# Key-value products of six batches in wider tiles, and fewer filler products, in a soft-MoE kernel over linear attention

## The reference

```python
kv  = einsum('bhsd,bhse->bhde', k, v)             # per batch and head: 64x64
out = einsum('bhsd,bhde->bhse', q, kv)
x   = out / sqrt(mean(out*out, -1) + 1e-6) * g_norm   # then (4608, 512)
logits = x @ phi                                   # (4608, 32)
d = exp(logits - logits.max(0)); d /= d.sum(0) + 1e-9
slot_input = (d.T @ x)                             # 32 slots
slot_out[e] = relu(slot_input[e] @ w1[e]) @ w2[e]  # w1: 512x1024, w2: 1024x512
c = exp(logits - logits.max(1)); c /= c.sum(1) + 1e-9
return c @ slot_out                                # (4608, 512)
```

## Time and profile before

| | |
|---|---|
| median of the runs | 171.85 us |
| profiled execution, its span | 172.24 us, 170.8 us |
| TensorE busy | 148.4 us (87%), 1821 matmuls and as many weight loads |
| VectorE, ScalarE, GpSimd busy | 85.7, 89.0, 60.6 us |
| DMA | 71.65 MB, 419 GB/s over the span |
| mean granted clock of TensorE | 0.975 of full speed |

### The profile page before, as it was taken

How to read it: one execution, slowest core, us unless ns; L and a number is a source line. 1 busy time by engine, 2 the same in 40 slices (tenths; PEclk the granted TensorE clock), 3 DMA queues, 4 the chain that set the end, 5 groups by cost and what they waited for, 6 DMA issues and landing times.

```text
span 170.8 us, 4205 instructions
## 1 busy us (share of the span) xinstructions
PE 148.4 (87%) x1821; PEld 103.4 (61%) x1821; DVE 85.7 (50%) x184; ACT 89.0 (52%) x232; POOL 60.6 (36%) x76
## 2 busy tenths in 40 slices
PE   7978998979999999999899998899989799988100
PEld 3547887969767878797697673366557443445000
DVE  1111437743669166762946698636885046229100
ACT  3114778795887686859749866213221044328100
POOL 7000246757177735477382678700000004000000
PEclk9999999999999999999999999999999999999955
DMA  5999999999999999999899999999999989999995
GB/s 183 436 450 407 482 411 419 430 502 414 414 405 468 414 444 479 418 429 418 384 420 465 460 426 395 470 412 387 418 430 445 455 387 414 429 413 430 423 452 236
DMA packets 3357, 71.65 MB, mean 419 GB/s; under 512 B 678, under 2 KB 678, under 8 KB 810
## 3 DMA queue, kind: packets, MB, share of 16 engines
q1 hardware_dynamic: 2986, 71.18, 97.4%
q0 software_dynamic: 352, 0.20, 0.4%
HBM read 61.94 MB, written 9.44 MB: 418 GB/s over the span
## 4 chain that ended last, share of the span: by engine, by line
PE 43%; DMA 31%; ACT 10%; DVE 6%; SPq 1%; issue 1%
PE psum L205 43%; DMA arena<-in_kv_dram 20%; DMA arena<-in_w_dram 11%; ACT bd L205 3%; ACT sq L205 2%; ACT arena L205 2%; DVE ms L205 2%; DVE logits L205 1%; SPq L205 1%; ACT part L205 1%; ACT d L205 1%; DVE part L205 1%; ACT r L205 1%; DVE acc L205 0%; DVE r L205 0%
## 5 line engine op out<-in xcount | busy, mean ns | idle before, releaser
L205 PE MATMUL psum<-bd,arena 128*128 128x192 f32 (+1 forms) x320 | 56.8, 336 | 2.2 <-ACT arena L205 1.0
L205 PEld LDWEIGHTS psum<-bd,arena 128*128 128x128 f32 (+1 forms) x320 | 45.5, 179 | 10.5 <-ACT arena L205 3.5
L205 PE MATMUL psum<-arena 128*64 128x64 f32 (+2 forms) x896 | 36.0, 270 | 2.9 <-DMA arena<-in_kv_dram 1.8
L205 DVE TENSOR_REDUCE ms<-sq 128x16 f32<-128x1024 f32 (+1 forms) x19 | 22.0, 1162 | 29.9 <-ACT sq L205 29.7
L205 PEld LDWEIGHTS psum<-arena 128*64 128x64 f32 (+2 forms) x896 | 27.5, 129 | 13.8 <-issue 4.1
L205 POOL TENSOR_TENSOR part<-part,r 128x512 f32<-128x512 f32 x17 | 17.8, 1047 | 49.7 <-DVE r L205 49.7
L205 POOL TENSOR_TENSOR arena<-arena,r 128x512 f32<-128x512 f32 x34 | 34.7, 1042 | 0.0
L205 ACT COPY arena<-psum 128x512 f32<-128x512 f32 (+2 forms) x48 | 30.8, 651 | 7.1 <-PE psum L205 7.1
L205 ACT ACTIVATE sq<-psum 128x512 f32<-128x512 f32 x36 | 21.5, 596 | 9.5 <-PE psum L205 9.3
L205 ACT COPY part<-psum 128x256 f32<-128x256 f32 (+1 forms) x38 | 13.7, 360 | 10.5 <-DVE part L205 9.3
L205 DVE TENSOR_REDUCE logits<-part 128x64 f32<-128x512 f32 (+1 forms) x17 | 17.2, 1013 | 0.0
(11 more groups left out here) (75 smaller groups left out, 103.4 us busy)
## 6 DMA issues: line engine op xcount, KB each, us to landing
arena<-in_kv_dram SPq DMA_DIRECT2D x1, 6912.0 KB, 30.4
arena<-in_t_dram SPq DMA_DIRECT2D x1, 6912.0 KB, 25.2
arena<-in_w_dram SPq DMA_DIRECT2D x1, 6912.0 KB, 28.0
arena<-in_w_dram SPq DMA_DIRECT2D x1, 6144.0 KB, 24.2
arena<-in_w_dram SPq DMA_DIRECT2D x3, 2048.0 KB, 18.8
arena<-in_w_dram SPq DMA_DIRECT2D x1, 5120.0 KB, 18.6
arena<-in_w_dram SPq DMA_DIRECT2D x1, 4352.0 KB, 31.8
arena<-in_w_dram SPq DMA_DIRECT2D x1, 4096.0 KB, 23.3
```

Source lines behind the costliest of these rows:

```text
L205: inst = getattr(engine, method)(*args, **kwargs)
```

## The change

Batches 0 to 4 (`WIDE = 5`) get a PSUM area twice as wide, a 128x128 block for each pair of heads. In batch 0 every product of 128 tokens, and that of the last 64, is taken for two heads at once: one 128x128 matmul in place of two of 64x64, of which the two 64x64 blocks on the diagonal are used. In batches 1 to 4 only the last 64 tokens are taken so, and first (with `start`); the 64x64 products of the main chunks add to the diagonal blocks. `kvT` is then copied in two halves of 64 partitions, for batch 0 one on ScalarE and one on VectorE, for batches 1 to 4 both on ScalarE. Batches 5 to 7 stay. The filler products ahead of the loop go from five products of zeros and two of ones to one and three; in each half of batch 0 one product of zeros goes, and behind the first half there is one of ones in place of two.

```diff
-EARLY = (5, 2, 0)
+EARLY = (1, 1, 0)
...
+WIDE = 5
...
+            if self.wide:
+                half = kv_rest(self.b, g).rearrange("p (w n) -> p w n", w=2)[64 * w : 64 * w + 64]
+                nc.tensor.matmul(
+                    self.pkv[:, w, g], lhsT=half[:, 1], rhs=half[:, 0], start=g == 0 or self.b == 0, stop=False
+                )
             for c in range(4):
+                if self.b == 0:
+                    nc.tensor.matmul(
+                        self.pkv[:, w, g], lhsT=main[:, w, 1, c], rhs=main[:, w, 0, c], start=False, stop=c == 3
+                    )
+                    continue
                 for i in range(2):
                     lo = 64 * i
+                    at = lo if self.wide else 0
                     nc.tensor.matmul(
-                        self.pkv[lo : lo + 64, w, g],
+                        self.pkv[lo : lo + 64, w, g, at : at + 64],
...
-            for g in gs:
+            for g in () if self.wide else gs:
...
-            nc.scalar.copy(self.kvT, self.pkv[:, :, gs[0] : gs[0] + n].rearrange("p w g d -> p g w d"))
+            pkv = self.pkv[:, :, gs[0] : gs[0] + n].rearrange("p w g d -> p g w d")
+            if not self.wide:
+                nc.scalar.copy(self.kvT, pkv)
+                return
+            nc.scalar.copy(self.kvT[:64], pkv[:64, :, :, :64])
+            if self.b:
+                nc.scalar.copy(self.kvT[64:], pkv[64:, :, :, 64:])
+            else:
+                nc.vector.tensor_copy(out=self.kvT[64:], in_=pkv[64:, :, :, 64:])
...
-    fill_wide(ps.tile([P, 512], F32, tag="m", name="fill"), 2)
+    fill_wide(ps.tile([P, 512], F32, tag="m", name="fill"), 3)
...
         kv.borders((g,))
-        fill(1, cols=512)
         kv.slots((g,))
```

More of the change, by code:

```diff
@@ L390, in __init__ @@
             t = ps.tile([P, 2, 512], F32, tag=tag, name=f"kvp{b}_{tag}", bufs=bufs)
-            self.pkv = t[:, :, :128].rearrange("p w (g d) -> p w g d", g=2)
-            self.pT = t[:, 0, 128:384].rearrange("p (g n) -> p g n", g=2)
-            self.pM = t[:, 1, 128:384].rearrange("p (g h w n) -> p g h w n", g=2, h=2, w=2)
+            self.wide = b < WIDE
+            n = 256 if self.wide else 128
+            self.pkv = t[:, :, :n].rearrange("p w (g d) -> p w g d", g=2)
+            self.pT = t[:, 0, n : n + 256].rearrange("p (g n) -> p g n", g=2)
+            self.pM = t[:, 1, n : n + 256].rearrange("p (g h w n) -> p g h w n", g=2, h=2, w=2)
         def products(self, r):
@@ L397, in products @@
             main = kv_main(self.b, g).rearrange("p (r w c n) -> p r w c n", r=2, w=2, c=4)
-            for c in range(4):
+            if self.wide:
[3 more added lines that the diff above has]
+                )
+            for c in range(4):
+                if self.b == 0:
[3 more added lines that the diff above has]
+                    continue
                 for i in range(2):
                     lo = 64 * i
+                    at = lo if self.wide else 0
                     nc.tensor.matmul(
-                        self.pkv[lo : lo + 64, w, g],
+                        self.pkv[lo : lo + 64, w, g, at : at + 64],
                         lhsT=main[:, w, 1, c, lo : lo + 64],
                         rhs=main[:, w, 0, c, lo : lo + 64],
-                        start=c == 0 and (g == 0 or self.b == 0),
-                        stop=False,
+                        start=c == 0 and g == 0 and not self.wide,
+                        stop=self.wide and g == 1 and c == 3,
                     )
         def borders(self, gs):
-            for g in gs:
+            for g in () if self.wide else gs:
                 half = kv_rest(self.b, g).rearrange("p (w n) -> p w n", w=2)
```

## The result

The changed kernel takes 178.91 us (median of 6 runs, 178.43 to 179.39) beside 171.84 of the kernel before on the same chip (171.59 to 171.95): a ratio of 1.0414, interval 1.0393 to 1.0434. The forecast was 171.5. The profiled execution took 179.14 with a span of 177.8, 7.0 more than before. Two executions at a far lower clock, of 191.41 us (kernel before) and 709.93 us (last experiment), are left out of all times, but the fetches of the last experiment are counted in the latter. The wide batches are five, 0 to 4, not six as the title has it.

The account below looks back on a forecast made before the run. The prediction took the last DMA engine to bound the kernel: one fetch fewer gains 0.35 us, TensorE's added time costs nothing, so 171.85 becomes 171.50 us. Forecast 171.35 to 171.65; wider range 171.2 to 171.95.

Parts of the forecast that it names:

- What bounds the kernel: Whole span: DMA engines stream 71.65 MB at 430 GB/s without a hole; the last engine to finish ends the kernel.
- How late could a DMA be: Loads and last store: slack is time from issue to landing less own bytes at 430 GB/s; 8.7, 6.4, 1.6 us.
- 8.7 us to spare: Load of `in_t`, 6912 KB: 25.2 us to landing against 16.5 us for its bytes.
- 6.4 us: Slack of the 5120 KB of weights that tile 35's stage releases: 18.6 us to landing against 12.2 for the bytes.
- 1.6 us for the last store: Slack of the last store, 3072 KB: 4.2 us beyond its bytes, of which some 2.6 are what any DMA pays.
- TensorE's time: Batches 0 to 4: fewer instructions but more TensorE time, 0.85 us per half of batch 0, 0.75 per later batch; costs nothing.
- At most 3.9 us late at the weights' issue: TensorE's delay bound there: up to 2.4 us passed on from batches 0 to 2, plus 1.5 from batches 3 and 4.
- The path of the delay: Batches 0 to 2 add up to 3.2 us; idling before the fourth batch's load takes 0.76; batches 3 and 4 add 1.5.
- Fetches: TensorE's instruction queue: 156 instructions fewer, so the fourteenth 16 KB fetch, at 154.67 us, falls away; gain 0.35 us.
- no gain: Rival, 171.85 us: the fetch is not on the last DMA engine, or comes all the same; chance 0.16.
- Slower: Rival, from 172.2 to 174 us: TensorE late at the last store, 1.4 us at the bound; chance 0.07.
- clock branch: Part of the slower rival: TensorE's clock falls around 10 us with fewer fillers, some 5 us of hole.

Follow-up runs that it names:

- last experiment: Kernel before with five products of ones exchanged for 32 tiny products of zeros each, meant to bring one fetch more (15); 172.07 us, ratio 1.0033.
- delay behind the issue: Kernel before with two more products of ones (1.7 us of TensorE) directly behind the issue of the last weights; 171.75 us, ratio 0.9997.
- batch 0 alone: Changed kernel with only batch 0 wide, batches 1 to 4 as in the kernel before; 171.97 us, ratio 1.0002.
- batches 1 and 2 in one row, tiny products: Batches 0 to 2 wide, wide products grouped, with 32 tiny products of zeros for one product of ones ahead of batch 0; 172.06 us, ratio 1.0013.
- batches 1 and 2 in one row: Changed kernel, batches 0 to 2 wide: wide products of 1 and 2 ahead of the narrow, batch 0's 64-row products side by side; 172.01 us.
- same with zeros thinned: Wide products of batches 1 and 2 grouped as in its parent, with fewer zero products, 32 TensorE instructions fewer; 172.40 us, ratio 1.0053.
- short delay: Kernel before with two more products of ones in front of tile 14, TensorE 1.7 us later; 173.19 us, ratio 1.0068.
- batches 1 to 3 in one row, copy on VectorE: Batches 0 to 3 wide, wide products grouped, second half of the transposed keys and values copied by VectorE, zeros thinned; 173.17 us, ratio 1.0092.
- all batches in one row, tiny products: Changed kernel with each batch 1 to 4's wide products grouped and 32 tiny products of zeros for one product of ones; 173.46 us, ratio 1.0090.
- all batches in one row: Changed kernel with the four wide products of each of batches 1 to 4 together ahead of the narrow ones; 173.30 us, ratio 1.0084.
- long delay: Kernel before with five more products of ones in front of tile 14, TensorE 4.3 us later; 174.77 us, ratio 1.0164.
- batches 1 to 4 alone: Changed kernel with batch 0 and all fillers as in the kernel before, batches 1 to 4 wide; 177.61 us, ratio 1.0349.

## Why the prediction was wrong

The delay of the last weights' issue (in the profiled execution, beside 106.10 of before) and the time added (ratio less 1, times 171.8):

| run | issued late, us | added, us |
|---|---|---|
| delay behind the issue | 0.10 | -0.05 (-0.2 to 0.1) |
| batch 0 alone | 0.16 | 0.03 (-0.2 to 0.2) |
| batches 1 and 2 in one row, tiny products | 0.41 | 0.2 (0.0 to 0.4) |
| batches 1 and 2 in one row | 0.52 | 0.2 (0.0 to 0.4) |
| same with zeros thinned (lower clock in eight of nine) | 0.54 | 0.9 (0.3 to 1.5) |
| short delay | 1.37 | 1.2 (0.8 to 1.5) |
| batches 1 to 3 in one row, copy on VectorE | 1.72 | 1.6 (1.2 to 2.0) |
| all batches in one row, tiny products | 1.87 | 1.5 (1.3 to 1.8) |
| all batches in one row | 2.21 | 1.4 (1.2 to 1.7) |
| long delay | 3.95 | 2.8 (2.6 to 3.1) |
| batches 1 to 4 alone | 6.23 | 6.0 (5.6 to 6.4) |
| changed kernel | 7.90 | 7.1 (6.8 to 7.5) |

*What bounds the kernel: right.* The DMA engines do. The two runs with the load's issue in place (0.10 and 0.16 late) keep the time, one of them with 1.7 us of work put on TensorE behind it.

*How late could a DMA be: wrong, and by itself enough to miss the forecast.* The prediction's "8.7 us to spare" and "6.4 us" came from the time to landing less the bytes at the mean rate. A landing is that of the last of 16 engines; the first to run dry decides. In the kernel before, the first 40 KB packet of these weights begins 3.1 us behind its issue (109.21), and where the engines already wait it takes 0.95 (114.95 less 114.00 in the changed kernel). That gave 2.2 us, and the short delay showed less. At 1.37 late two engines end their packets at 109.13 and 109.39, and the two packets of these weights that do not follow another packet's end within 10 ns begin at 110.32 and 110.46, the first 2.85 us behind the issue. So two engines lose about 1.1 us each. The last engine ends at 171.34 in place of 170.34, while the mean of the 16 is only 0.3 later; that it is one of these two is likely, as each engine has its own share of a load, but no record names the engines. Between 0.5 and 1.4 us the delay begins to cost, and from there on it costs 0.65 to 0.97 of its length. Even the delay that the prediction allowed, 3.9 us, costs 2.8 by the long delay. The 8.7 us for `in_t` were too many as well: 6.05 late, it left the hole at 52 us. The 1.6 us for the last store no run tests.

*TensorE's time: the sign right, one term missing, the sum wrong by two.* "At most 3.9 us late at the weights' issue" was 7.9, "2.2 us" for a half of batch 0 was 3.08, "0.38 us later" for a batch was 1.71. The paces of the passes were about right: in one row the products cost 0.25. What the prediction put at nothing, without a reason, is the alternation of wide and narrow: 0.49 us for each beyond the first, three a batch, which is 5.9 us for four batches, and 0.6 in each half of batch 0. The Trainium skill, "TensorEngine Tiling (Array Packing)", section "Key Properties", says that a change of tiling mode, other than a move to another tile, drains TensorE; the runs fit this, at the price above, and the prediction did not weigh it. What is shown is that the order costs; whether a drain, the weight loads at the change of shape or the write into the same part of PSUM behind the wide product is the cause, these runs don't tell apart. *The path of the delay* is as the prediction had it: batch 0's by itself is absorbed, and the wait at 37.48 takes up to 0.8. The rest adds up: 1.48 at batch 1's start (0.49 more than with batch 0 alone; in that execution batch 0 itself began later, at 6.91, not 6.42), less 0.76, with 1.71 for each of batches 1, 2 and 4 and 1.57 for batch 3, is 7.4. The half copies of `kvT` put 0.14 a batch on it: from the next products with the queries to `ident,kvT` 0.90 us go by, not 0.76. (The prediction allowed up to 0.37.) That makes 8.0, where 7.9 were measured.

*Fetches: the count right, the worth not.* Thirteen in place of fourteen, as 256 instructions to a block said; the last at 157.7, not 148, with the rest of the kernel late. (Where a stream ended just short of a mark, as with batches 1 and 2 in one row, the closing instructions brought a fetch all the same.) The gain of 0.35 us is not seen: with 13 fetches and the load 0.54 late one engine still ended 0.67 behind the next, and 15 at the clock of before took no longer than 14, within 0.1 us. That the engine with the fetch is the one that ends last was a reading of one execution; the rival "no gain" named that doubt, and no run shows that the fetch sets the end. Whether it is worth 0.1 us stays open.

*The rivals.* "Slower" came, at 0.07 of the chances. Its place was wrong: the last store, where it was a load; so was its price, bounded by 1.4. Its clock branch did not come: the granted clock is 1.00 from 10 to 164 us.

*What stays open.* No version here beats the kernel before. Why late loads have longer packets is not shown, and these are 2.9 of the 7.1 us. The run with batch 3 and thinned zeros shows no hole of the size of its 1.6 us; some of that may be the thinning.

## What to carry to other kernels

Where the DMA queues are full, as here, a load has no more slack than the engine that runs dry first; the time to landing less the bytes at the mean rate is no measure of it. A delay of known length, put ahead of its issue and then behind it, shows in two runs whether the slack is shorter than the delay. Count a product's cost with its neighbours, not by its passes alone: of the orders tried here, products of one tile shape together were the cheapest. Fewer instructions can be more time.

## What was not expected of the hardware

A load issued 1.37 us late, and 1.7 us ahead of the time at which the first engine came to it before (109.21), still left two engines without work for about a microsecond. The packets of late loads took longer, those of the stores behind them did not. With fewer zero products the mean clock was lower in some executions only: thinned out by 14 pairs of weight load and matmul, eight of nine runs had 0.940 to 0.958 where the kernel before has 0.968 to 0.978, and exchanged for tiny ones, six of eleven had 0.952 to 0.967. No profile shows in which stretch.
